# An order of steps in a sparse attention and mixing kernel: two transposes ahead of the last projection, the exponential and its biases at the end of a slot

## What is computed

```python
scores = (q @ k^T) / sqrt(64)                     # 4 batches, 8 heads, 576 tokens, 64 wide
kth    = 32nd largest score of each row
attn   = exp(scores - max) where scores >= kth, else 0;  attn /= sum(attn) + 1e-9
x      = attn @ v, heads side by side             # (4, 576, 512)
gate   = sigmoid(causal 5-tap convolution of x along the tokens, per channel)
x      = (gate * (x @ w_val)) @ w_out
mixed  = real(fft over tokens and over channels of x)
u      = x + mixed
un     = (u - mean(u)) / sqrt(var(u) + 1e-6)      # per token, over 512 channels
out    = u + relu(un @ w_ch1) @ w_ch2             # 512 -> 2048 -> 512
```

## Time and profile before

| | us |
|---|---|
| median of 3 runs | 1212.93 |
| lowest and highest | 1212.51 and 1215.17 |
| the profiled execution, whole | 1214.56 |
| its span in the trace | 1212.8 |
| TensorE busy | 1049.4 |
| VectorE busy | 884.3 |
| ScalarE busy | 621.3 |
| GpSimd busy | 406.9 |

### The profile page before, as it was taken

How to read it: one execution, slowest core, us unless ns; L and a number is a source line. 1 busy time by engine, 2 the same in 40 slices (tenths; PEclk the granted TensorE clock), 3 DMA queues, 4 the chain that set the end, 5 groups by cost and what they waited for, 6 DMA issues and landing times.

```text
span 1212.8 us, 19844 instructions
## 1 busy us (share of the span) xinstructions
PE 1049.4 (87%) x6608; PEld 841.9 (69%) x6608; DVE 884.3 (73%) x1898; ACT 621.3 (51%) x1253; POOL 406.9 (34%) x704
## 2 busy tenths in 40 slices
PE   3776565789798989989798989999798999998998
PEld 2554454666587878866587878775587888648887
DVE  6999999996996978696996978696996970330000
ACT  3786766644565655554565655454565653012221
POOL 2444533142443332233433332322443322133221
PEclk9886756889898999999898999999898999998999
DMA  8566455021355856321355846321365655206974
GB/s 256 163 202 203 140 187 188 11 74 35 102 209 193 282 192 198 134 75 46 111 217 192 270 178 213 123 70 45 126 226 202 226 179 204 108 1 237 351 277 162
DMA packets 81188, 200.37 MB, mean 165 GB/s; under 512 B 8384, under 2 KB 26560, under 8 KB 81088
## 3 DMA queue, kind: packets, MB, share of 16 engines
q1 hardware_dynamic: 81088, 199.11, 48.2%
HBM read 177.58 MB, written 21.50 MB: 164 GB/s over the span
## 4 chain that ended last, share of the span: by engine, by line
PE 56%; issue 14%; DVE 12%; POOL 10%; ACT 5%; DMA 1%; SPq 1%; DVEq 0%; ACTq 0%; POOLq 0%
PE p_m L567 15%; PE p_m L553 15%; PE p_m L461 14%; DVE rest L742 5%; PE p_t L434 4%; PE p_t L450 4%; PE p_s L421 4%; DVE top L748 3%; ACT prob L630 2%; POOL k_lo L876 2%; POOL bias L884 1%; POOL hid_lo L949 1%; POOL w_st L901 1%; POOL bias L885 1%; DMA u<-w_ch 1%
## 5 line engine op out<-in xcount | busy, mean ns | idle before, releaser
L748 DVE MAX8 top<-rest 128x8 f32<-128x576 f32 x432 | 304.7, 747 | 0.0
L949 POOL TENSOR_TENSOR hid_lo<-hid,hid_hi 128x256 fp32r<-128x256 f32 (+1 forms) x128 | 107.0, 836 | 325.8 <-ACT hid_hi L692 325.8
L742 DVE MATCH_REPLACE8 rest<-top,rest 128x576 f32<-128x576 f32 x288 | 211.7, 743 | 0.0
L553 PE MATMUL p_m<-un_hi,w_st 128*128 128x320 f32 (+1 forms) x1024 | 172.9, 313 | 44.6 <-POOL un_lo L940 25.3
L567 PE MATMUL p_m<-w_st,hid_hi 128*128 128x512 f32 x640 | 206.3, 404 | 0.2 <-POOL hid_lo L949 0.2
L553 PEld LDWEIGHTS p_m<-un_hi,w_st 128*128 128x128 f32 x1024 | 149.6, 198 | 55.5 <-POOL un_lo L940 26.2
L630 ACT ACTIVATE prob<-s_sb,bias 128x576 f32<-128x576 f32 x144 | 111.1, 772 | 105.0 <-POOL bias L885 104.6
L623 ACT ACTIVATE s_sb<-p_s 128x576 f32<-128x576 f32 x144 | 93.1, 646 | 136.3 <-PE p_s L421 136.2
L434 PE MATMUL p_t<-id_sb,prob 128*128 128x128 f32 x720 | 122.1, 306 | 34.4 <-ACT or_sb L652 34.0
L421 PE MATMUL p_s<-k_hi,q_st 128*128 128x512 f32 (+1 forms) x320 | 118.2, 372 | 33.2 <-POOL k_lo L876 19.5
L450 PE MATMUL p_t<-pT,v_sb 128*64 128x128 f32 (+1 forms) x1600 | 106.9, 285 | 43.5 <-ACT pT L643 23.4
(11 more groups left out here) (78 smaller groups left out, 1602.9 us busy)
## 6 DMA issues: line engine op xcount, KB each, us to landing
w_st<-w_split SPq DMA_DIRECT2D x256, 512.0 KB, 4.4
w_split<-w_st SPq DMA_DIRECT2D x32, 512.0 KB, 3.0
q_raw<-qT SPq DMA_DIRECT2D x64, 144.0 KB, 3.4
k_raw<-kT SPq DMA_DIRECT2D x64, 144.0 KB, 3.4
u<-w_ch SPq DMA_DIRECT2D x32, 256.0 KB, 3.6
v_sb<-v SPq DMA_DIRECT2D x16, 256.0 KB, 3.5
wslot<-w_val SPq DMA_DIRECT2D x4, 1024.0 KB, 5.3
wslot<-w_out SPq DMA_DIRECT2D x4, 1024.0 KB, 5.3
```

What stands on the lines that cost most here:

```text
L553: mm = pe.matmul(mbank(HIDDEN_BANK[g], n), w1_st[i % NB1][:, w, k, :], x[:, k, at:at + n], start=part + k == 0, stop=part + k == KC + 1)
L742: dve.match_replace(rest[tt % 2][:, :], top[tt % 4][:, 8 * n - 8:8 * n], src[:, :], LOWEST).then_inc(s_chain, 1)
L748: found = dve.max(top[tt % 4][:, 8 * n:8 * n + 8], rest[tt % 2][:, :])
L949: pool.tensor_tensor(hid_lo[i % 2][:, 0:WIDTH[g]], hid[:, 0:WIDTH[g]], hid_hi[i % 2][:, 0:WIDTH[g]].bitcast(F32), ALU.subtract).then_inc(m ...
```

## The change

Three things move, and no instruction is added or removed.

1. In `STEPS` the transposes of the first token group (`trn 0`, `trn 1`) come ahead of `seq 2` and of `proj 4`. They fall in slots 88 and 89 instead of 89 and 90 (and likewise in the other batches), `proj 4` in 90 instead of 89. `normalise` of the two tiles moves to `proj 1` and `proj 2`.
2. On ScalarE `exponent(s-4)` is the last of the slot instead of ahead of the steps.
3. On GpSimd `biases(s-4)` is the last of the slot instead of ahead of the steps.

```diff
--- before.py
+++ after.py
@@ -66,13 +66,13 @@
 
 
 STEPS = [("val", j) for j in range(2 * KC)] + [("zed", m) for m in (2, 0, 1)]
-STEPS += [("seq", 0), ("proj", 0), ("proj", 1), ("seq", 1), ("proj", 2), ("proj", 3), ("seq", 2), ("trn", 0), ("proj", 4),
-          ("trn", 1)]
+STEPS += [("seq", 0), ("proj", 0), ("proj", 1), ("seq", 1), ("proj", 2), ("proj", 3), ("trn", 0), ("seq", 2), ("trn", 1),
+          ("proj", 4)]
 for f in range(FC + 1):
     STEPS += [("ch0", f)] + ([("trn", f // 3 + 1)] if f in (3, 6, 9) else [])
 STEPS += [("ch1", f) for f in range(FC + 1)]
 
-NORM_AT = {("proj", 2): 0, ("seq", 2): 1, ("ch0", 1): 2, ("ch0", 4): 3, ("ch0", 7): 4}
+NORM_AT = {("proj", 1): 0, ("proj", 2): 1, ("ch0", 1): 2, ("ch0", 4): 3, ("ch0", 7): 4}
 COST = {"val": 2.2, "zed": 3.5, "seq": 2.6, "proj": 3.5, "trn": 0.6, "ch0": 3.1, "ch1": 3.7}
 
 SELECT, EXPONENT, RECIP, TRANSPOSE, ATTEND = 1, 4, 6, 6, 7
@@ -701,8 +701,6 @@
                     if split_due(s) is not None:
                         split_high(split_due(s), 0)
                         split_high(split_due(s), 1)
-                    if due(s, EXPONENT):
-                        exponent(s - EXPONENT)
                     if part_due(s) is not None:
                         split_weights(part_due(s))
                     if s in FEAT_SLOTS:
@@ -717,6 +715,8 @@
                         gate_tanh(b, c)
                     for x in plan[s][1:]:
                         step(*x)
+                    if due(s, EXPONENT):
+                        exponent(s - EXPONENT)
 
             @block.vector
             def _(dve):
@@ -954,8 +954,6 @@
                 for s in plan:
                     if split_due(s) is not None:
                         split_low(split_due(s))
-                    if due(s, EXPONENT):
-                        biases(s - EXPONENT)
                     if part_due(s) is not None:
                         split_weights(part_due(s))
                     for x in plan[s][0:1]:
@@ -964,6 +962,8 @@
                         scale_out(s - ATTEND)
                     for x in plan[s][1:]:
                         step(*x)
+                    if due(s, EXPONENT):
+                        biases(s - EXPONENT)
 
         numbers = sorted(x.num for x in sems)
         assert numbers == list(range(numbers[0], numbers[-1] + 1))
```

## The result

The changed kernel takes 1298.15 us in the median of 4 runs (1296.11 to 1299.08), beside 1213.55 of the kernel before in the same session (1212.51 to 1215.17): ratio 1.069, 95% interval 1.0675 to 1.0712. The forecast of 1234 had the direction and a quarter of the size, and the range ended at 1252. The profiled execution has a span of 1296.7 us, 83.9 more than before.

What follows compares the result with a forecast made beforehand. VectorE was taken to bound the first 251 us, TensorE the overlapped batches. Batches of +4.7, +7.3 and +12.5 and the last's -2.7 gave +21.8 on a span of 1212.8: median about 1234, eight in ten between 1212 and 1252.

Steps and rivals of the forecast that it cites:

- In the first 251 us VectorE bounds: First stage, slots up to about 43: its even selection needs a bias ready 0.9 to 4 us before, so 0.
- The third rival: Slower still: in the first stage VectorE's selection waits for a late bias, one us in each of 21 rounds: 1255, chance 10%.
- Values, +6.8: Second batch, slots 79 to 83: late bias and exponential make attend wait for `pT`, slot 83 starts 6.8 us later.
- Projections and transposes, +6.9: Second batch, slots 83 to 91: late deviation, bias and `make_u` delay the first hidden step by 6.9 us.
- The step list: Transposes moved ahead of `proj 4`: alone, exponential as before, the first hidden step comes forward by about 4 us.
- Pair boundaries, -5.6 and -5.2: Channel steps of both groups, second batch: evacuation no longer behind the bias, waits of 4.70 and 3.13 us and slow stretches go.
- slow stretch: TensorE matmuls at about half clock after a wait; waits that go give it back, waits that come bring one.
- Smaller terms, +4.4: Channel steps, second batch: attend waits 2.1 us (0.4 before), twice, and three small waits make 1.0; +4.4 us.
- Batches: The three overlapped batches, all terms together: first +4.7, second +7.3, third +12.5 us.
- The last batch, -2.7: Last batch, without attention: hidden starts 0.9 us after `proj 4`, at 1090.9 and not 1093.65, -2.7 us.
- Sum: Whole kernel: all terms together +21.8 us on a span of 1212.8, giving 1234.6.

Runs made afterwards that it cites:

- early to proj: Changed kernel with the biases early in slots 0 to 43 and in slots with a val, zed, seq, proj or trn step: 1204.47 us, ratio 0.991.

## Where the prediction was right and where it was wrong

- **The step that failed: "In the first 251 us VectorE bounds; its even selection needs a bias that by the same count is ready 0.9 to 4 us before ...: 0."** It measured +46.0 by slot 43. The count asked in one round whether the bias came before the selection that wants it, and took the old starts of that round. But the edit had closed a round: exponential behind bias, bias behind split or scale_out, those behind `pT`, `pT` behind the exponential of the slot before. Then the question is not who is late in a slot but how long one turn takes. It can be added up from durations of before: 5.5 and 7.4, 12.9 a pair against VectorE's 10.1 to 10.6 (with every attend at full speed 11.8, which is still more). The third rival had the place and priced it as one slipped us a round, 21 in all, with a chance of 10%; it is 2.9 us in each pair of slots between 18 and 33 (13.5 against 10.6 by the score copies at 121.3 and 222.4, and at 98.2 and 177.8, pair boundaries included).
- **Values, +6.8**: the mechanism and its hand count hold. Attend of slot 80 stood 5.67 (6.0 predicted), slot 82's 3.51; the term measured +8.3 (+8.4 by slot 84).
- **Projections and transposes, +6.9**: attend in the third projection's slot stood 3.40 (3.7 predicted), and VectorE's `u` (ends 667.5), not `un_lo`, is the last thing before the first hidden step. From the first score matmul of slot 79 to that step it is 108.9 us against 92.3, +16.6 for both terms where I had 13.7. By the score copies of slots 83 and 91, +8.9.
- **The step list**: alone it should bring that step about 4 forward. It brought it 0.5 forward, counted from slot 79: the wait of 7.20 was taken for time to be won, but `proj 4` moves into it. That it gained 17 us in all comes mainly from the clock, behind this wait and a later one, and from the last batch.
- **Pair boundaries, -5.6 and -5.2**: the waits of 4.70 and 3.13 are gone, and none of TensorE's waits there exceeds 1.5. Slots 98 to 99 give -4.5, 107 to 110 -2.8. The second was over-sized: with the biases early the same three slots give -6.0, so the late bias takes half of it back. Its 2.8 us of slow stretch are not tied to the wait either: with the step list alone the wait of 3.13 stays and the stretch is gone.
- **Smaller terms, +4.4** measured +6.0 a batch (+4.4, +0.7 and +0.9). The two attends stood 2.19 each, with 2.1 predicted. In a channel step `hid_lo`, bias and exponential stand one behind the other, and VectorE's selection waits behind the same bias (4.10 at 694.86), which my sum left out.
- **Batches**: +11.4, +15.8 and +16.9 where I had 4.7, 7.3 and 12.5, the second too small by 1.5 in the values, 2.0 in the projections, 3.5 at the boundaries and 1.6 in the channel steps.
- **The last batch, -2.7 "and up to 2.4 more if the slow stretch goes"**: -6.1. It goes; the wait there is 0.96, and the windows of before and after have a clock of 0.98 and 1.00 for the 229.4 and 223.3 us behind the last score copy.
- **Sum**: 37.9 behind slot 43 against 21.8, and 46.0 ahead of it against 0. Of the 62 us between forecast and span 46 are the one term that was set to nothing.

What the sum took with a wait, a slow stretch behind it, is seen for the attends of after behind 3.4 to 5.7 us of wait (2.40 us for 20 matmuls). Behind 2.19 us of wait at 705.2 the same 20 took 1.31, and behind 2.18 at 988.4 they took 2.40. The 8 matmuls of the first hidden step took 2.04 behind a wait of 3.73 in after, and 1.19 behind one of 3.70 in `early to proj`. The rule of the Trainium skill ("TensorE: Matmul & The Clock Gate", Part 1), that the throttled state is the default and activity releases it, agrees with the slow ones; the others show that not each wait brings a slow stretch, and that its length alone doesn't tell.

What stays open: what decides whether a wait of 2 to 4 us costs the clock; how much of the loss in the batches is the clock, which no run holds fixed; and what the two engines' blocking of each other, below, adds to it.

## What to carry to other kernels

When an edit moves an operation behind others in two in-order queues, look for a closed round through them and add up one turn of it from durations in the trace; compare it with the busiest engine's time for the same piece of work, in every stage, also where the moved operation had been no bottleneck. Putting the consumer last (the exponential) was worth 3.4%; putting its producer last too (the bias, 0.5 us of work for an engine busy a third of the time) cost 11%. A wait that an engine shows on a buffer can be an effect: doubling the buffers removed the wait, left the first stage as it was and gave back 10 of 84 us in the whole. And when stages are compared by a marker such as a score copy, look whether the same work lies on the same side of it in both kernels; the values' gain of 12 us was 8 once the next slot was counted in.

## What the runs showed of the hardware that I had not expected

In the first stage of after the granted clock is lower than before over the same slots: from slot 18 to 33 it was

```profile
121.30:222.40 101.10, 54.85 (x331) 45.14 (x331) 94.75 (x182) 55.83 (x106) 36.11 (x55) 0.61 0.44 144
```

and before, over 98.2 to 177.8, it was

```profile
98.20:177.80 79.60, 52.08 (x331) 43.65 (x331) 79.22 (x167) 55.94 (x106) 34.30 (x56) 0.65 0.57 186
```

With attends inside the round this matters as it didn't before. Between 95 and 222 us all 8 full-sized groups of attends in after take 2.4 us, the 1.2 GHz level, against 1.31 for the 20 matmuls at full speed; the two smaller ones, of a pair's last tile, take 1.33 where one of before took 0.80. So about 1.1 us of a slot's 7.44 is the clock, and by the groups up to slot 33 some 11 of the 44.6 us, an estimate. In before 7 of 10 full-sized groups ran at the same level, and VectorE was busy 239.5 of 251.3 us all the same.

VectorE and GpSimd do not meet by semaphores alone. VectorE's busy time is 33.8 us longer in after, 27 of it in two groups, here first before, then after:

```profile
L762 DVE TENSOR_TENSOR k_lo<-k_raw,k_hi 128x576 fp32r<-128x576 f32 x16 | 17.9, 1121 | 0.0
L771 DVE TENSOR_SCALAR rinv<-psum_row 128x2 f32<-128x2 f32 x72 | 17.4, 242 | 23.0 <-PE p_t L454 22.8 <-issue 0.3
...
L762 DVE TENSOR_TENSOR k_lo<-k_raw,k_hi 128x576 fp32r<-128x576 f32 x16 | 34.5, 2154 | 0.0
L771 DVE TENSOR_SCALAR rinv<-psum_row 128x2 f32<-128x2 f32 x72 | 27.5, 383 | 24.7 <-ACT prob L635 24.7
```

The shortest of L762 takes 0.74 us and of L771 0.15. The long ones end with an operation of GpSimd: L771 at 123.17 takes 1.25 and ends 0.03 behind GpSimd's piece of the split (123.11, 1.28), L762 at 53.75 takes 3.19 and ends 0.6 behind the second of two GpSimd operations in a row (L876 and L901). In before 5 of the 16 of L762 are long, in after 15. It goes the other way too: beside VectorE's convolution (L789, 149.00 to 151.68) the two bias operations take 0.60 and 0.85 us and not 0.22 and 0.30, and that slot's turn of the round is 6.40 and not 5.47. So a part of what counts as VectorE's busy time is waiting; no run here tells what it costs.
